# Adding a finished partial sum in PSUM before the last product instead of after it, and halving the last tile by rows

## The reference, cut to what matters

```python
def reference(...):
    x = attn(q, k, v, lam)                  # decayed linear attention, x is 1536 x 512
    h = x @ moe_w_in                        # 512 -> 2048
    y = np.maximum(0.01 * h, h) @ moe_w_out # 2048 -> 512
    a = y @ moe2_w1                         # 512 -> 1024
    b = y @ moe2_w2
    h = a * b @ moe2_w3                     # 1024 -> 1024
    return h @ moe2_w_out                   # 1024 -> 512
```

## Time and profile before

| what | us |
|---|---|
| median of 3 runs (510.79 to 511.63) | 511.36 |
| the profiled execution's own time | 510.73 |
| span of the profiled execution | 508.9 |
| TensorE busy | 504.7 (99%) |
| VectorE busy | 354.8 (70%) |
| ScalarE busy | 201.1 (40%) |

### The profile page before, as it was taken

How to read it: one execution, slowest core, us unless ns; L and a number is a source line. 1 busy time by engine, 2 the same in 40 slices (tenths; PEclk the granted TensorE clock), 3 DMA queues, 4 the chain that set the end, 5 groups by cost and what they waited for, 6 DMA issues and landing times.

```text
span 508.9 us, 9106 instructions
## 1 busy us (share of the span) xinstructions
PE 504.7 (99%) x3576; PEld 417.7 (82%) x3576; DVE 354.8 (70%) x536; ACT 201.1 (40%) x356; POOL 93.7 (18%) x102
## 2 busy tenths in 40 slices
PE   9999999999999999999999999999999999999997
PEld 7788888888888888888888888888888888888886
DVE  4677356867787866777665777597777745878962
ACT  5453353343456533333311546443333214473420
POOL 2232141112112321233300020323333300000000
PEclk9999999999999999999999999999999999999999
DMA  8999583344121111111000021212222115240012
GB/s 293 340 394 352 164 289 97 137 125 127 43 84 42 43 41 43 42 43 41 25 18 0 22 83 40 82 47 94 70 65 63 41 43 206 87 161 0 16 48 103
DMA packets 27065, 51.57 MB, mean 101 GB/s; under 512 B 4232, under 2 KB 4496, under 8 KB 27024
## 3 DMA queue, kind: packets, MB, share of 16 engines
q1 hardware_dynamic: 24560, 43.53, 25.6%
q10 hardware_dynamic: 2432, 7.47, 4.5%
q0 software_dynamic: 32, 0.00, 0.0%
HBM read 45.74 MB, written 5.25 MB: 100 GB/s over the span
## 4 chain that ended last, share of the span: by engine, by line
PE 98%; DMA 1%; ACT 0%; DVE 0%; SPq 0%; DVEq 0%; issue 0%
PE acc L1443 11%; PE acc L1444 11%; PE acc L1445 11%; PE hid L1644 10%; PE hid L1643 10%; PE hid L1645 10%; PE hid L1443 7%; PE hid L1445 7%; PE hid L1444 7%; PE hid L1472 1%; PE hid L1487 1%; PE acc L1771 1%; PE acc L1769 1%; PE acc L1770 1%; PE hid L1500 1%; PE hid L1511 1%
## 5 line engine op out<-in xcount | busy, mean ns | idle before, releaser
L1443 PE MATMUL acc<-g_hi,wb 128*128 128x512 f32 x224 | 87.6, 391 | 0.0
L1444 PE MATMUL acc<-g_lo,wb 128*128 128x512 f32 x224 | 87.2, 389 | 0.0
L1445 PE MATMUL acc<-g_hi,wb 128*128 128x512 f32 x224 | 87.2, 389 | 0.0
L716 POOL TENSOR_TENSOR w_in_lo_place<-stage 128x256 f32<-128x256 f32 x16 | 12.5, 784 | 211.6 <-PE hid L1645 121.6
L1443 PE MATMUL hid<-xy_hi,wa_hi 128*128 128x512 f32 x128 | 50.3, 393 | 0.0
L1445 PE MATMUL hid<-xy_hi,wa_lo 128*128 128x512 f32 x128 | 49.8, 389 | 0.0
L1444 PE MATMUL hid<-xy_lo,wa_hi 128*128 128x512 f32 x128 | 49.8, 389 | 0.0
L1643 PE MATMUL hid<-wa_hi 128*128 128x512 f32 x128 | 49.8, 389 | 0.0
L1644 PE MATMUL hid<-wa_lo,wa_hi 128*128 128x512 f32 x128 | 49.8, 389 | 0.0
L1645 PE MATMUL hid<-wa_hi,wa_lo 128*128 128x512 f32 x128 | 49.8, 389 | 0.0
L1443 PEld LDWEIGHTS acc<-g_hi,wb 128*128 128x128 f32 x224 | 42.0, 188 | 9.0
(11 more groups left out here) (222 smaller groups left out, 929.0 us busy)
## 6 DMA issues: line engine op xcount, KB each, us to landing
stage<-weights SPq DMA_DIRECT2D x109, 256.0 KB, 3.1
w_out_place<-attn ACTq DMA_DIRECT2D x12, 512.0 KB, 5.3
x_hi_place<-attn SPq DMA_DIRECT2D x4, 512.0 KB, 7.8
w_out_place<-attn SPq DMA_DIRECT2D x4, 512.0 KB, 7.7
w_dram<-x_lo_place SPq DMA_DIRECT2D x8, 256.0 KB, 5.1
stage<-w_dram SPq DMA_DIRECT2D x8, 256.0 KB, 2.7
x_lo_place<-attn SPq DMA_DIRECT2D x2, 512.0 KB, 5.9
x_hi_place<-attn ACTq DMA_DIRECT2D x2, 512.0 KB, 5.6
```

The source lines that it names most:

```text
L716: nc.gpsimd.tensor_tensor(s_1, a21, a22, ALU.add).then_inc(s_made, 1)
L1443: nc.tensor.matmul(out, w_hi, a_hi, start=first, stop=False)
L1444: nc.tensor.matmul(out, w_hi, a_lo, start=False, stop=False)
L1445: return nc.tensor.matmul(out, w_lo, a_hi, start=False, stop=final)
```

## The change

`u2` is added into Z's bank by VectorE before the last product accumulates onto it (`joined`), so that the bank holds the finished output when that product ends. TensorE waits for `joined` instead of `third_made`. After `pair_ready` 9, ScalarE copies the whole bank (VectorE added before), and SyncE stores it. After `pair_ready` 10, VectorE copies rows 0 to 63 of the last tile and SyncE stores them, while ScalarE copies rows 64 to 127 and stores them through its own queue. `half(i)` is rows 64i to 64i + 63; `WIDE` is 256 columns, `TOK` 512.

```diff
 # SyncE
-            wait_then_step(last_made, 1)
+            wait_then_step(third_tile_copied, 1)
             sp.dma_start(outT[0, :, tokens(2)], second_of_out(0)).then_inc(out_stored, 16)
-            wait_then_step(last_made, 2)
-            sp.dma_start(outT[1, :, 2 * TOK:2 * TOK + WIDE], second_of_out(1)[:, 0:WIDE]).then_inc(out_stored, 16)
+            wait_then_step(first_half_copied, 1)
+            sp.dma_start(outT[1, half(0), tokens(2)], second_of_out(1)[half(0), :]).then_inc(out_stored, 16)
 # ScalarE
-            act.wait_ge(last_made, 3)
-            act.dma_start(outT[1, :, 2 * TOK + WIDE:3 * TOK], second_of_out(1)[:, WIDE:TOK]).then_inc(tail_stored, 16)
+
+            act.wait_ge(pair_ready, 8 + 1)
+            nc.scalar.copy(second_of_out(0), bank(GATE_BANKS[0][0])).then_inc(third_tile_copied, 1)
+            act.wait_ge(pair_ready, 8 + 2)
+            nc.scalar.copy(second_of_out(1)[half(1), :], bank(GATE_BANKS[0][1])[half(1), :]).then_inc(second_half_copied, 1)
+            act.wait_ge(second_half_copied, 1)
+            act.dma_start(outT[1, half(1), tokens(2)], second_of_out(1)[half(1), :]).then_inc(tail_stored, 16)
 # VectorE
                 nc.vector.tensor_tensor(third_of_out(d), z_bank[d], third_of_out(d), ALU.add).then_inc(third_made, 1)
+
+                dve.wait_ge(third_made, 2 * d + 2)
+                dve.wait_ge(second_made, d + 1)
+                nc.vector.tensor_tensor(z_bank[d], z_bank[d], second_of_out(d), ALU.add).then_inc(joined, 1)
...
-            dve.wait_ge(pair_ready, 8 + 1)
-            nc.vector.tensor_tensor(second_of_out(0), z_bank[0], second_of_out(0), ALU.add).then_inc(last_made, 1)
             dve.wait_ge(pair_ready, 8 + 2)
-            for cols in (slice(0, WIDE), slice(WIDE, TOK)):
-                nc.vector.tensor_tensor(second_of_out(1)[:, cols], z_bank[1][:, cols], second_of_out(1)[:, cols],
-                                        ALU.add).then_inc(last_made, 1)
+            nc.vector.tensor_copy(second_of_out(1)[half(0), :], z_bank[1][half(0), :]).then_inc(first_half_copied, 1)
 # TensorE
             for d in range(2):
-                pe.wait_ge(third_made, 2 * d + 2)
+                pe.wait_ge(joined, d + 1)
                 out_product(z_bank[d], S4, B22, d, False)
```

More of the change, by code:

```diff
@@ L506, in build @@
         fourth_made = sem("fourth_made")
-        last_made = sem("last_made")
+        joined = sem("joined")
+        third_tile_copied = sem("third_tile_copied")
+        first_half_copied = sem("first_half_copied")
+        second_half_copied = sem("second_half_copied")
         t_made = sem("t_made")
```

## The result

| | before | changed |
|---|---|---|
| median of 18 runs each, us | 511.37 | 512.62 |
| lowest to highest | 510.65 to 512.29 | 511.89 to 514.39 |
| the profiled execution's own time | 510.73 | 513.94 |
| its span | 508.9 | 512.2 |
| last matmul's end to the span's end ("the tail") | 2.92 | 4.20 |

The change makes the kernel slower by 1.25 us: the ratio is 1.0029 (95% interval 1.0021 to 1.0037). The two profiled executions differ by 3.2 us, more than the medians. So executions are compared here by their tail, from the last matmul's end (its start + 0.39) to the span's end. It grew by 1.28 us, near the 1.25 of the medians.

A forecast was written before the change was run, and what follows sets the result against it. TensorE, 98% of the 508.9 us span, was taken to bound the kernel. TensorE cost 0 and last landing 508.59 against 508.60 left the span at 508.9, own time 510.7, median 511.3 us, range 510.8 to 511.9.

The forecast's parts named there:

- TensorE and the sums into Z's bank: Before the last products: each of two added VectorE sums takes 0.69 us, and TensorE does not wait for them.
- The cost of 0: At TensorE's waits before the last products: the added sums delay it by 0, with 1.05 us of slack at the tightest.
- The rival of a dear PSUM sum: Sums written into PSUM: slow enough that TensorE waits, 512.5 us at 2.8 us a sum; chance 2%.
- The last tile's copies: Behind the last matmul: 64-row copies take 0.68 us on VectorE and 0.58 on ScalarE, time going by columns.
- The rival of turns: Last tile: the two copies of one bank run one after the other, 0.51 us later, 511.9 us; chance 3%.
- Third tile: Third tile: ScalarE's copy takes 0.58 us instead of VectorE's sum of 0.69; the store 0.1 us earlier gives nothing.
- The two stores: End of the kernel: same bytes in longer rows, flow about 0.78 us, last landing at 508.59 against 508.60.
- the half-rate case: Last stores: halves with 64 rows move at half the rate, flow 1.56 us instead of 0.78, +0.8 us; chance 5%.
- The range of +0.2 at the top: Upper bound on the change's summed effect on time, the lower bound being -0.3 us.
- slow half stores: Last tile's stores of 64 rows move at half the rate, +0.8 us, 512.1 us; chance 5%.

The follow-up runs named there:

- e4: The changed kernel, but with the last tile copied by VectorE in two column halves and stored in two column halves, as before; 511.44 us, ratio 1.0000.
- g4: f1 with 8 empty instructions at the head of both VectorE's and ScalarE's programs; 512.27 us, ratio 1.0023.
- g1: The changed kernel with 8 empty instructions at the head of VectorE's program; 511.80 us, ratio 1.0008.
- e1: The kernel before, with the last tile stored as two row halves (64 x 512), both issued once both column sums are done; 512.45 us, ratio 1.0020.
- e2: The kernel before, with the first column store of the last tile held back so both column stores are issued at once; 511.57 us, ratio 1.0001.
- g2: The changed kernel with 8 empty instructions at the head of ScalarE's program; 512.79 us, ratio 1.0020.
- f1: The changed kernel, copies by rows kept, but the last tile stored in two column halves once both copies are done; 512.82 us, ratio 1.0028.
- g3: The kernel before with 2 empty instructions at the head of each of VectorE's and ScalarE's programs; 512.40 us, ratio 1.0018.
- f2: The kernel before, with the last tile stored as two row halves, both issued by SyncE after both column sums; 512.57 us, ratio 1.0024.
- f3: The kernel before, with two earlier tiles stored in pieces of 64 or 32 rows, each waited for, some 24 us before the end; one execution, tail 2.92 us.

## Why the prediction was wrong

The forecast was no change at 511.3 us, 96% within 0.2%; it came out at 512.62, outside the range of 510.8 to 511.9, slower than before by 1.25 us (0.24% by the medians, 0.29% by the ratio).

What held, by the steps of the prediction:
- *TensorE and the sums into Z's bank*: 0.70 us against 0.69, `joined` in time, the first sum on `g` on its matmul. The cost of 0 is confirmed by e4. The rival of a dear PSUM sum fell.
- *The last tile's copies*: time goes by columns, 0.68 and 0.58 as forecast, side by side. The rival of turns fell (g4). The issues came 0.64 and 0.80 us behind the last matmul's end, forecast 0.65 and 0.81.
- *Third tile*: 0.59 us, no effect.

What failed is the step *The two stores*. It took bytes and row length for all that sets a store's time, and read "the flow is bound by bytes" out of stores that all had 128 rows. Two terms were wrong:
1. The cut by rows. The prediction added, from the first issue on, 0.82 until the data flow, 0.78 of flow and 0.35 to the landing. In g1, where the fetch is away, these are 1.2, 1.1 and 0.3: the lead and the flow are each some 0.35 us longer than they were put. Against the kernel before (tail 2.92, g1 3.72) the 0.80 us are 0.1 of a later first issue (0.65 behind the last matmul instead of 0.55), 0.4 of lead, 0.2 of flow and 0.1 that is left behind the landing. I gave the half-rate case 5% and priced it at +0.8, but by a flow of 1.56 us, which no run shows for the two stores of a changed kernel: only the first of them is slow. That its price is g1's 0.80 is luck. The lead of 0.82 was taken over from stores of 128 rows without a reason. e1 against e2, at equal issue times, gives the shape alone 0.42; e2 against before gives 0.53 for sending both column halves at the later moment, and there the landing took 2.0 and 2.2 us when both queues issued together, against 1.8 when they were 0.27 apart.
2. A term that the sum did not have: the place of the last instruction fetch. It is 4.20 - 3.72 = 0.48 us here, 0.77 by g2 (4.49) against g1, 0.71 by f1 (4.16) against g4 (3.45), and 1.07 by g3 (3.99) against before (2.92). The medians would give it more of the loss, 1.25 - 0.27 = 0.98 us, and the rows 0.27; with their scatter of 0.4 us and one profile for each tail, how the loss divides is known only roughly. That both parts are there is not in doubt: e1 has the rows without the fetch, g3 the fetch without the rows. The prediction counted instructions' time, not their number. The range of +0.2 at the top would have had to hold +1.3.

The rival "slow half stores" alone, 512.1, plus this term, 0.5, is the measured 512.6, but this is the same luck. Of the rule on disjoint halves I took that they serialize, and not what one half alone does to the rate. Two small slips changed nothing: 507.31 to 508.25 is 0.94 us of flow and not 0.90, and the dear sum at 2.8 us gives 512.4 and not 512.5.

Open is why the issue of a 64-row store is 0.2 us longer than those of 32 and 128 rows and its data come 0.3 to 0.4 us later; why the second half store flows at some 400 GB/s behind one on another queue (e1, g1) and at half of that on the same queue (f2) or alone (f3); why the same fetch costs 0.5 us in one tail and 1.1 in another. The foot, at the rate of one engine of 16, suggests one DMA engine late by 0.2 to 0.7 us, but in g3 it ends at 510.1 and the store lands at 508.53 + 2.9 = 511.43, so some of the delay lies behind the last data packet, and the records do not show on what. Open too is why the place goes by the length of VectorE's whole program, as e4 shows, whose extra instruction comes after the fetch.

## What to carry to other kernels

Cut the last tile so that each store spans all 128 partitions: by columns, the first piece sent ahead, not by rows. A sum moved ahead of the last product saves nothing where the copy that stays takes as long as the sum. When a difference under 1 us at the end of a kernel has no cause in the arithmetic, look for an instruction fetch among the last packets, and add a few empty instructions early on to see whether it goes.

## What the runs showed of the hardware that I had not expected

- Four empty instructions at the head of two programs cost 0.87 us at the end (g3). Eight took 0.48 us off the tail of the changed kernel and left +0.27 instead of +1.25 in the medians. In both a fetch of 8 KB moved. The Trainium skill (Runtime: NRT & Kernel Launch, Instruction fetch mechanics) calls the cost of such a crossing mostly hidden and the block 16 KiB; here queue 14 moves 8 KB a time (14 packets, 0.11 MB), queue 8 16 KB (28 packets, 0.46 MB), and at the end it costs 0.5 to 1.1 us.
- 128 KB from rows 0 to 63 flow alone in some 0.65 us, from rows 32 to 95 in 0.45 (f3); behind a store of rows 64 to 127 on the other queue rows 0 to 63 flow at some 400 GB/s too (e1, g1). The issue takes 0.49 to 0.59 us for 64 rows and 0.33 to 0.38 for 32 or 128, and the data follow 1.2 us behind it instead of 0.8 to 0.9.
- VectorE adds into a PSUM bank in place in 0.70 us, and matmuls accumulate onto what it wrote.
